# Two of three matrix products by Strassen's scheme, four stages with DRAM between them, cosine by half angle

## The chip, the cores and the metric

One core of a Trainium2 chip runs the whole program. The metric is the device time of one execution in microseconds (us), median of several runs. Every operand is float32. A product at near float32 precision is made of three TensorE passes over rounded operands (type float32r): high by high, high by low, low by high, where "low" is what the rounding of "high" left over.

## The reference, cut to what matters

```python
B, H, S, D = 4, 8, 768, 64        # 3072 tokens of 8 x 64 = 512 values
# attention: chunks of 32 queries; keys: 8 memory rows, 16 left, 32 own, 8 right
scores = (q_c @ k_full.T) / 8;  a = softmax(scores);  out_c = a @ v_full
x = out as [3072, 512]
h = x @ w_in                      # [512, 2048]
x = (h * cos(h)) @ w_out          # [2048, 512]
h = max(x @ w1, x @ w2, x @ w3)   # each [512, 768]
result = h @ w_out2               # [768, 512]
```

## The kernel before, in words

Attention runs on 24 subblocks of 128 tokens. For one of them TensorE makes the scores (L324, 16 small matmuls), VectorE subtracts the maximum (L616, L620), ScalarE takes the exponential of three subblocks at once (L486, after a load of its function table), TensorE turns the probabilities (L337), ScalarE copies them out (L493), TensorE multiplies with the values (L350), VectorE divides by the sum (L643), TensorE turns the result (L358), and ScalarE and VectorE write its high and low part (L497, L649).

The two expert layers run on 8 blocks of 384 tokens. **Stage 1** does attention, first product, cosine and second product together. For each of 16 slices f of the 2048 hidden features, `hidden` makes 12 matmuls of 384 columns (4 slices of 128 inputs, 3 passes), and `second` adds the slice that lies three behind it (LAG) into the output, 12 matmuls more. The attention of the next block stands between them by a fixed rule on f (`attend`). Between the products a slice is copied out of PSUM and turned into an angle on ScalarE (L504, L506), reduced to the range of the sine on VectorE (L662, L668, L677), passed through the sine on ScalarE (L512), multiplied and split in high and low on VectorE (L665, L674, L680). All weights of the stage stay in SBUF: POOL loads them once (L282) and subtracts for the low part (L287), after ScalarE rounded the high part (L531). The result goes to DRAM (`y_dram`), 768 KB a block.

**Stage 2** reads it back (L522, L690 for high and low), and for 6 slices of 128 features makes three products of 12 matmuls (`branch`), takes the largest of the three (L594, L755, L758), splits it (L764, L766), and `project` multiplies by the last matrix: 9 matmuls of 512 columns, summed over the 6 slices.

In numbers: 1536 + 1536 + 1728 matmuls of 384 columns and 432 of 512 columns. Each engine runs its own list in order, semaphores tie the lists together, and steady blocks are hardware loops (`blocks`). The loads of the attention come from SP's queue into one buffer for queries and keys and one for values: each load waits until the matmuls of the subblock before have read the buffer (L184).

Of the kernel before, what the change touches and what calls it, by code (L numbers as in the profile page):

```python
# [5 lines left out]
F32 = mybir.dt.float32  # L6
F32R = mybir.dt.float32r
I32 = mybir.dt.int32
# [8 lines left out]
P = 128  # L17
SUB = 128
NCH = SUB // CH
PAIRS = H // 2  # L20
BLK = 384
NSUB = BLK // SUB
NBLK = B * S // BLK
SUBS = B * S // SUB
# [9 lines left out]
LAG = 3  # L34
AHEAD = 3
WARM = 8
WSLOTS2 = NM * (NB2 + 1) // 2


PI = 3.141592653589793  # L40
ROUND = 1.5 * 2.0 ** 23
GONE = -3.0e38


def program(nc, qk_in, v_in, w1_in, w2_in, y_dram, out):
    ctx = ExitStack()
    with ctx:
# [6 lines left out]

        wts = sb("wts", [P, NF, 2, 2, 512], F32R)

        xh = sb("xh", [P, 2, KT, BLK], F32R)
        xl = sb("xl", [P, 2, KT, BLK], F32R)

        gh = sb("gh", [P, 4, BLK], F32R)  # L60
        gl = sb("gl", [P, 4, BLK], F32R)
        stage_and_tiles = sb("stage_and_tiles", [P, 8 * BLK])
        ostage = stage_and_tiles[:, 0:4 * BLK]
        tiles = stage_and_tiles[:, 4 * BLK:8 * BLK]
        hid = tiles[:, 0:2 * BLK].rearrange("p (b t) -> p b t", b=2)
        ang = tiles[:, 2 * BLK:4 * BLK].rearrange("p (b t) -> p b t", b=2)

        qk = sb("qk", [P, PAIRS * (2 * KC + SUB)])  # L70
        vals = sb("vals", [P, PAIRS * 2 * KC])
        prob = sb("prob", [P, NSUB, PAIRS, 2, KEYS])
        prob_t = sb("prob_t", [P, PAIRS, SUB])
        onat = sb("onat", [P, PAIRS, 2, D])
# [4 lines left out]
        wraw = sb("wraw", [P, 2, 2, 512])  # L79
        ident = sb("ident", [P, P])  # L80
        half_pi = sb("half_pi", [P, 1])
# [3 lines left out]
        yout = ostage[:, :].rearrange("p (m t) -> p m t", m=KT)  # L85
        ofin = ostage[:, 0:NSUB * DM].rearrange("p (i n) -> p i n", i=NSUB)
        yin = qk[:, 0:KT * BLK].rearrange("p (m t) -> p m t", m=KT)

        spare = stage_and_tiles[:, 0:PAIRS * (2 * KC + SUB)]

        def qk_at(t, j):
            b = spare if (t is T0 and j == 1) else qk[:, :]
            return b.rearrange("p (a x) -> p a x", a=PAIRS)

        def queries(t, j):
            return qk_at(t, j)[:, :, KC:KC + SUB]

        def keys(t, j, a, c):  # L100

            return two_parts(qk_at(t, j), a, c, KC + SUB)

        def vals_at(t, j):


            return (spare if (t is T0 and j == 1) else vals[:, :]).rearrange("p (a x) -> p a x", a=PAIRS)

        def head1_at(t, j):
            return KC + SUB if (t is T0 and j == 1) else KC  # L110

        def values_in(t, j, a, c):
            return two_parts(vals_at(t, j), a, c, head1_at(t, j))
# [6 lines left out]
        ps = ctx.enter_context(nc.psum_tensor("ps", [P, 8, 512], F32))  # L120
        T0 = 0
        HB = (4, 5)
        WB = (6, 7, 4, 5)

        def scores(t, j):
            return ps[:, (7, 5, 1)[j] if t is T0 else 7, :].rearrange("p (a r k) -> p a r k", a=PAIRS, r=2)

        def turned(t, j):
            return ps[:, (6, 4, 0)[j] if t is T0 else 6, :].rearrange("p (a t) -> p a t", a=PAIRS)

        def weighted(t, j):
            return ps[:, (7, 5, 1)[j] if t is T0 else 7, :].rearrange("p (a r d) -> p a r d", a=PAIRS, r=2)

        def inputs_at(n):


            return 32 * n

        def block_at(t):

            return t + NSUB

        qk_landed, v_landed = sem("qk_landed"), sem("v_landed")
        qk1_landed, v1_landed, zeroed = sem("qk1_landed"), sem("v1_landed"), sem("zeroed")
        w_landed = [sem("w_landed0"), sem("w_landed1")]
        w_high, w_ready = sem("w_high"), sem("w_ready")
        const_ready, const_base = sem("const_ready"), sem("const_base")
        qk_done, edge_masked, max_done, shifted = sem("qk_done"), sem("edge_masked"), sem("max_done"), sem("shifted")
# [4 lines left out]
        h_done, h_copied, turns_done = sem("h_done"), sem("h_copied"), sem("turns_done")  # L153
        k_done, r_done, abs_done, cos_done = sem("k_done"), sem("r_done"), sem("abs_done"), sem("cos_done")
        g_done, gh_done, g_ready, y_done = sem("g_done"), sem("gh_done"), sem("g_ready"), sem("y_done")
        y_out_act, y_out_dve, y_stored, y_landed = sem("y_out_act"), sem("y_out_dve"), sem("y_stored"), sem("y_landed")
        yh_ready, y_ready = sem("yh_ready"), sem("y_ready")
        br_done, first_copied, second_maxed, third_maxed = (
            sem("br_done"), sem("first_copied"), sem("second_maxed"), sem("third_maxed"))
        mh_done, m_ready, o_done = sem("mh_done"), sem("m_ready"), sem("o_done")  # L160
        fin_act, fin_dve, out_stored = sem("fin_act"), sem("fin_dve"), sem("out_stored")
# [4 lines left out]

        def blocks(eng, one):

            one(0, 0, True, False)
            with eng.Fori(0, (NBLK - 2) // 2) as i:  # L170
                one(2 * i + 1, 1, False, False)
                one(2 * i + 2, 0, False, False)
            one(NBLK - 1, (NBLK - 1) % 2, False, True)


        @block.sync
        def _(sp):


            def split_load(src, buffer, n, columns, landed):  # L180

                for r in range(2):
                    rows = slice(P // 2 * r, P // 2 * (r + 1))
                    sp.dma_start(buffer[rows, :, columns[r]],  # L184
                                 src[bass.ds(n, 1), rows, :].rearrange("n p (a x) -> (n p) a x", a=PAIRS))\
                      .then_inc(landed, 16)

            QK_COLUMNS = (slice(0, KC + SUB), slice(KC, 2 * KC + SUB))

            def v_columns(t, j):  # L190
                return (slice(0, KC), slice(head1_at(t, j), head1_at(t, j) + KC))

            def load_qk(n):
                sp.wait_ge(qk_done, n)
                sp.wait_ge(const_ready, 1)
                split_load(qk_in, qk_at(None, 0), n, QK_COLUMNS, qk_landed)

            def load_v(n):
                sp.wait_ge(pv_done, n)
                sp.wait_ge(const_ready, 1)  # L200
                split_load(v_in, vals_at(None, 0), n, v_columns(None, 0), v_landed)

            def store_y(t):

                sp.wait_ge(y_out_act, 2 * t + 2)
                sp.wait_ge(y_out_dve, 2 * t + 2)
                sp.wait_ge(const_ready, 1)
                sp.dma_start(y_dram[bass.ds(t, 1), :, :].rearrange("n p c -> (n p) c"), ostage).then_inc(y_stored, 16)
# [12 lines left out]

            def loads1(t, more, store):


                n = NSUB * t
                for j in range(1, NSUB + more):
                    load_qk(n + j)
# [591 lines left out]
```

## Time and profile before

| | |
|---|---|
| median of 3 runs | 1081.99 us (1080.62 to 1083.03) |
| span of the profiled execution | 1079.6 us |
| TensorE matmuls busy | 1032.5 us, 96% |
| VectorE, ScalarE, GpSimd busy | 538.5, 330.7, 83.6 us |
| DMA | 66.05 MB, mean 61 GB/s |
| mean granted TensorE clock | 0.983 of full speed |

The span runs from the first to the last instruction, the device time some 2 us longer. The durations of matmuls overlap, so that the distance between two starts, and not the duration, tells what one costs. Stage 1 lasts until some 680 us, stage 2 from there on.

### The profile page before, as it was taken

The numbers are of one execution on the slowest core, as the hardware profiler recorded it, in microseconds if no ns is written. First come the engines' busy times: TensorE is split into PE (matmuls) and PEld (weight loads), VectorE is DVE, ScalarE is ACT, GpSimd is POOL, SyncE is SP. The second block draws the span as 40 slices with busy tenths as digits, with TensorE's granted clock in tenths as the row PEclk, the third lists the DMA queues.
The fourth block names the chain that finished last, engine by engine and source line by source line (L and its number), as shares of the span: only waits on it lengthen the run. The fifth ranks groups of instructions, "written<-read, shape, count | busy, mean of one in ns | idle before, by whom it ended". The sixth has DMA issues, their size and how long they took to land.

```text
span 1079.6 us, 17509 instructions
## 1 busy us (share of the span) xinstructions
PE 1032.5 (96%) x6976; PEld 984.1 (91%) x6976; DVE 538.5 (50%) x1132; ACT 330.7 (31%) x575; POOL 83.6 (8%) x64
## 2 busy tenths in 40 slices
PE   5797999999999999999999977999999999999998
PEld 4687999999999999999999976999999999999997
DVE  5576665665665666665665666323222322233222
ACT  2455354344353353353443443101110101101000
POOL 1554000000000000000000354000000000000000
PEclk7699999999999999999999999999999999999999
DMA  8743231241321321311320231201010000000000
GB/s 212 183 143 117 69 89 40 52 107 30 73 77 40 89 49 42 101 39 40 89 59 11 70 97 59 85 4 59 3 58 30 29 29 29 29 29 29 0 30 30
DMA packets 35722, 66.05 MB, mean 61 GB/s; under 512 B 2368, under 2 KB 26944, under 8 KB 35648
## 3 DMA queue, kind: packets, MB, share of 16 engines
q1 hardware_dynamic: 31616, 50.34, 16.9%
q0 software_dynamic: 4032, 14.68, 4.2%
q8 instruction: 52, 0.85, 0.3%
q14 instruction: 22, 0.18, 0.1%
HBM read 52.43 MB, written 12.58 MB: 60 GB/s over the span
## 4 chain that ended last, share of the span: by engine, by line
PE 84%; DVE 8%; ACT 5%; DMA 2%; issue 1%; SPq 0%; ACTq 0%; DVEq 0%
PE ps L305 23%; PE ps L307 23%; PE ps L306 23%; DVE stage_and_tiles L662 3%; PE ps L461 3%; PE ps L462 3%; PE ps L460 3%; PE ps L350 2%; PE ps L324 2%; ACT wts L531 2%; DMA qk<-qk_in 1%; DVE stage_and_tiles L668 1%; ACT stage_and_tiles L506 1%; PE ps L358 1%; ACT stage_and_tiles L504 1%
## 5 line engine op out<-in xcount | busy, mean ns | idle before, releaser
L305 PE MATMUL ps<-xh,wts 128*128 128x384 f32 x1088 | 375.2, 345 | 3.1 <-issue 1.7
L307 PE MATMUL ps<-xh,wts 128*128 128x384 f32 x1088 | 366.6, 337 | 0.0
L306 PE MATMUL ps<-xl,wts 128*128 128x384 f32 x1088 | 365.9, 336 | 0.0
L305 PEld LDWEIGHTS ps<-xh,wts 128*128 128x128 f32 x1088 | 205.8, 189 | 14.7 <-issue 10.8
L306 PEld LDWEIGHTS ps<-xl,wts 128*128 128x128 f32 x1088 | 206.1, 189 | 2.0
L307 PEld LDWEIGHTS ps<-xh,wts 128*128 128x128 f32 x1088 | 205.7, 189 | 0.0
L305 PE MATMUL ps<-gh,wts 128*128 128x384 f32 x512 | 172.2, 336 | 13.1 <-DVE gl L680 12.8
L662 DVE TENSOR_SCALAR stage_and_tiles<-stage_and_tiles 128x384 f32<-128x384 f32 x128 | 76.6, 598 | 212.8 <-ACT stage_and_tiles L506 212.8
L307 PE MATMUL ps<-gh,wts 128*128 128x384 f32 x512 | 171.4, 335 | 0.0
L306 PE MATMUL ps<-gl,wts 128*128 128x384 f32 x512 | 171.1, 334 | 0.0
L512 ACT ACTIVATE stage_and_tiles<-stage_and_tiles,half_pi 128x384 f32<-128x384 f32 x128 | 79.0, 617 | 237.2 <-DVE stage_and_tiles L677 237.1
L755 DVE TENSOR_TENSOR stage_and_tiles<-stage_and_tiles,ps 128x384 f32<-128x384 f32 x48 | 26.6, 554 | 201.3 <-PE ps L307 201.3
L594 ACT COPY stage_and_tiles<-ps 128x384 f32<-128x384 f32 x48 | 23.1, 482 | 305.5 <-PE ps L307 305.5
L305 PEld LDWEIGHTS ps<-gh,wts 128*128 128x128 f32 x512 | 96.2, 188 | 16.6 <-DVE gl L680 16.0
L287 POOL TENSOR_TENSOR wts<-wraw,wts 128x1024 fp32r<-128x1024 f32 x28 | 66.7, 2381 | 566.5 <-ACT wts L531 566.5
L306 PEld LDWEIGHTS ps<-gl,wts 128*128 128x128 f32 x512 | 96.1, 188 | 0.0
L307 PEld LDWEIGHTS ps<-gh,wts 128*128 128x128 f32 x512 | 96.1, 188 | 0.0
L504 ACT COPY stage_and_tiles<-ps 128x384 f32<-128x384 f32 x128 | 61.3, 479 | 102.6 <-PE ps L307 102.6
L506 ACT ACTIVATE stage_and_tiles<-ps,rounder 128x384 f32<-128x384 f32 x128 | 75.0, 586 | 0.0
L665 DVE TENSOR_TENSOR stage_and_tiles<-stage_and_tiles 128x384 f32<-128x384 f32 x128 | 70.4, 550 | 0.2 <-ACT stage_and_tiles L512 0.2
L668 DVE SCALAR_TENSOR_TENSOR stage_and_tiles<-stage_and_tiles 128x384 f32<-128x384 f32 x128 | 70.4, 550 | 0.0
L680 DVE TENSOR_TENSOR gl<-stage_and_tiles,gh 128x384 fp32r<-128x384 f32 x128 | 70.3, 550 | 0.0
(63 smaller groups left out, 828.3 us busy)
## 6 DMA issues: line engine op xcount, KB each, us to landing
qk<-qk_in SPq DMA_DIRECT2D x46, 384.0 KB, 5.1
wraw<-w_in POOLq DMA_DIRECT2D x28, 512.0 KB, 3.7
vals<-v_in SPq DMA_DIRECT2D x46, 256.0 KB, 3.8
y_dram<-stage_and_tiles SPq DMA_DIRECT2D x8, 768.0 KB, 6.3
qk<-y_dram SPq DMA_DIRECT2D x8, 768.0 KB, 4.3
out<-stage_and_tiles SPq DMA_DIRECT2D x8, 768.0 KB, 3.6
stage_and_tiles<-qk_in SPq DMA_DIRECT2D x2, 384.0 KB, 9.2
stage_and_tiles<-v_in SPq DMA_DIRECT2D x2, 256.0 KB, 6.2
```

What stands on the lines that cost most here:

```text
L287: pool.tensor_tensor(wts[:, s, :, 1, :], wraw[:, g % 2, :, :], wts[:, s, :, 0, :].bitcast(F32), ALU.subtract).then_inc(w_ready, 1)
L305: pe.matmul(o, wh, mh, start=start, stop=False)
L306: pe.matmul(o, wh, ml, start=False, stop=False)
L307: return pe.matmul(o, wl, mh, start=False, stop=stop)
L460: pe.matmul(o, gh[:, m % 3, toks], w[:, 0, :], start=(m == 0), stop=False)
L504: act.copy(hid[:, f % 2, :], ps[:, HB[f % 2], 0:BLK]).then_inc(h_copied, 1)
L506: act.activation(ang[:, f % 2, :], ps[:, HB[f % 2], 0:BLK], ACT.Identity, scale=1.0 / (2 * PI), bias=rounder[:, :]).then_inc(turns_done, 1)
L512: act.activation(a, a, ACT.Sin, scale=-1.0, bias=half_pi[:, :]).then_inc(cos_done, 1)
L662: dve.tensor_scalar(a, a, ROUND, None, ALU.subtract).then_inc(k_done, 1)
L665: dve.tensor_tensor(hp, hp, ap, ALU.mult).then_inc(g_done, 1)
L668: dve.scalar_tensor_tensor(out=a, in0=a, scalar=-2 * PI, in1=hid[:, f % 2, :], op0=ALU.mult, op1=ALU.add).then_inc(r_done, 1)
L680: dve.tensor_tensor(glp, hp, ghp.bitcast(F32), ALU.subtract).then_inc(g_ready, 1)
```

## The change

**Stages.** Stage 1 becomes two. In the first (here A) are attention and `hidden` only, in blocks of 384 tokens; the gated result g goes to DRAM (`g_dram`, 16 slices by 3072 tokens). In the second (B) g comes back and is multiplied by `w_out`. Stage 2 becomes two as well: the three products with their maximum, written to DRAM (C), and the last product (D).

**Strassen's scheme** (Winograd's form) in B, C and D: both operands are cut in four quarters, and 7 products of sums of quarters take the place of 8. The sums (4 subtractions or additions per operand and unit) are made from the unrounded quarters, and all 7 combinations are rounded and split in high and low. A unit of B (48 of them: 6 token blocks of 512, 8 pairs of feature slices) is 7 products of 2 x 3 = 6 matmuls of 256 columns. For it VectorE makes four sums of 256 columns (`sums_g`), ScalarE rounds 7 x 256 = 1792 columns (`high_g`), and VectorE subtracts 1792 columns (`low_g`). At the end of a block of 8 units VectorE joins the 7 products by 7 additions of 512 columns. A unit of C (36) is 42 matmuls of 384 columns; a unit of D (12) is 63 of 256 columns. D's other operand, the 18 groups h, is prepared like g.

**Cosine.** With u = h/2pi and r = round(u) - u, h cos h = 2pi u (1 - 2 sin²(pi r)). ScalarE now makes copy, angle, sine and square of two slices at once (768 columns), VectorE two operations (`turn`, `gated`). The factor -2pi goes into `w_out`.

**Buffers.** The whole program is written out, without loops. B's g has 2 raw buffers and 3 prepared ones. Queries and keys, and values, keep one buffer each in the steady blocks.

The diff, cut to its core:

```diff
-                    if f >= LAG:
-                        second(t, f - LAG, first)
+        def attend(t, f):
+            n = NSUB * (t + 1)
...
+                if f == 1:
+                    scores_of(n + 1)
+                elif f == 3:
+                    scores_of(n + 2)
+                elif f == 6:
+                    turn_probs(n)
...
+                elif f == 10:
+                    values(n + 1)
+                    turn_out(n)
+                elif f == 11:
+                    values(n + 2)
...
+                elif f == 15 and t < NBLK - 2:
+                    scores_of(n + NSUB)
...
+            for n in range(UNITS1):
+                b, i = divmod(n, FPAIRS)
+                pe.wait_ge(g_ready, n + 1)
...
+                g, w = operand(9 + n % 3), operand(i)
+                for p in ORDER1:
...
+            def evacuate(i):
...
+                act.activation(hid(i), hidden_banks(i), ACT.Copy, scale=1.0 / (2 * PI)).then_inc(u_copied, 1)
...
+                act.activation(ang(i), hidden_banks(i), ACT.Identity, scale=1.0 / (2 * PI), bias=rounder[:, :])\
...
+            def cosine(i):
+                act.wait_ge(r_done, i + 1)
+                act.activation(ang(i), ang(i), ACT.Sin, scale=BELOW_PI).then_inc(sin_done, 1)
+                act.wait_ge(sin_done, i + 1)
+                act.activation(ang(i), ang(i), ACT.Square, scale=ROOT_TWO).then_inc(square_done, 1)
...
+            for t in range(NBLK):
...
+                for f in range(NF):
...
+                    if f % 2:
+                        i = FPAIRS * t + f // 2
+                        evacuate(i)
+                        if i:
+                            cosine(i - 1)
...
+                        if f == 5:
+                            exps(0, NSUB, n + NSUB)
...
+            def sums_cols(r, done, base):
+                dve.tensor_tensor(r[:, 4, :], r[:, 1, :], r[:, 0, :], ALU.subtract).then_inc(done, 1)
+                dve.wait_ge(done, base + 1)
...
+                if n and n + 2 < UNITS1:
+                    sums_g(n + 2)
+                if i == FPAIRS - 1:
...
+                    dve.tensor_tensor(y12, y11, ps[:, BANK1[6], :], ALU.add).then_inc(u2_done, 1)
...
+                if n and n + 2 < UNITS1:
+                    low_g(n + 2)
...
+            for n in range(UNITS1):
+                if n % FPAIRS == 0 and n:
+                    store_y(n // FPAIRS - 1)
...
+                if n >= 2 and n + 2 < UNITS1:
+                    load_g(n + 2)
...
+HIGH_H = (32, 33, 34, 35, 36, 37, 38, 38, 39, 40, 40, 41, 42, 42, 43, 44, 44, 45)
...
+                if 1 <= n <= 7:
+                    low_w2(n + 1)
...
+                for r in range(HUNITS):
+                    if HIGH_H[r] == n:
+                        sums_h(r)
+                for r in range(HUNITS):
+                    if HIGH_H[r] == n:
+                        low_h(r)
```

In the last lines n is the unit of C and D that TensorE works on; ScalarE's list has `high_w2(n + 1)` and `high_h(r)` at the same places. TensorE's list for a unit is products 1, 5, 7 (of the unit before), 2, 6, 3, 4 (of the unit before).

**Where instructions move, first place:** ScalarE in the first block, around the exponential of the attention. Before (`stage_and_tiles` holds the copied slice and the angle):

```order
L504 COPY stage_and_tiles<-ps 128x384
L506 ACTIVATE stage_and_tiles<-ps,rounder 128x384
L486 ACT_TABLE_LOAD
L486 ACTIVATE prob<-prob 128x1536
L512 ACT_TABLE_LOAD
L512 ACTIVATE stage_and_tiles<-stage_and_tiles,half_pi 128x384
```

And after, in the second block (`work` holds the slices, the angles and the probabilities):

```order
L805 ACTIVATE work<-ps 128x768
L808 ACTIVATE work<-ps,rounder 128x768
L813 ACTIVATE work<-work 128x768
L815 ACTIVATE work<-work 128x768
L784 ACT_TABLE_LOAD
L784 ACTIVATE work<-work 128x1536
L790 COPY prob_turned<-ps 128x512
```

The exponential now stands behind the sine and the square of the slice pair before.

**Second place:** VectorE in the second product. Before, for one slice:

```order
L662 TENSOR_SCALAR stage_and_tiles<-stage_and_tiles 128x384
L665 TENSOR_TENSOR stage_and_tiles<-stage_and_tiles 128x384
L668 SCALAR_TENSOR_TENSOR stage_and_tiles<-stage_and_tiles 128x384
L674 CAST gh<-stage_and_tiles 128x384
L677 TENSOR_SCALAR stage_and_tiles<-stage_and_tiles 128x384
L680 TENSOR_TENSOR gl<-stage_and_tiles,gh 128x384
```

After, the last unit of a block of B (`work` is the raw g and the sums of the result, `units` the prepared operands; L1084 to L1090 are `sums_g`, L1099 is `low_g`):

```order
L1084 TENSOR_TENSOR work<-work 128x256
L1086 TENSOR_TENSOR work<-work 128x256
L1088 TENSOR_TENSOR work<-work 128x256
L1090 TENSOR_TENSOR work<-work 128x256
L1228 TENSOR_TENSOR work<-work,ps 128x512
L1231 TENSOR_TENSOR work<-work,ps 128x512
L1099 TENSOR_TENSOR units<-work,units 128x1792
L1236 TENSOR_TENSOR work<-work,ps 128x512
L1238 TENSOR_TENSOR work<-work 128x512
L1240 TENSOR_TENSOR work<-work 128x512
L1243 TENSOR_TENSOR work<-work,ps 128x512
L1246 TENSOR_TENSOR work<-work,ps 128x512
```

In the other units the four sums stand directly ahead of `low_g`, which waits for ScalarE's `high_g` of the same unit, and that waits for the sums.

**Third place:** VectorE in the last product. Before, for one slice of the hidden features, it had this:

```order
L755 TENSOR_TENSOR stage_and_tiles<-stage_and_tiles,ps 128x384
L758 TENSOR_TENSOR stage_and_tiles<-stage_and_tiles,ps 128x384
L764 CAST gh<-stage_and_tiles 128x384
L766 TENSOR_TENSOR gl<-stage_and_tiles,gh 128x384
```

After, one unit of D (L1278 `c22` of the unit before, L1294 `c11`, L1299 `c12`), with two groups of h behind it:

```order
L1278 TENSOR_TENSOR work<-work,ps 128x256
L1294 TENSOR_TENSOR work<-work,ps 128x256
L1299 TENSOR_TENSOR work<-work,ps 128x256
L1132 TENSOR_TENSOR work<-work 128x256
L1134 TENSOR_TENSOR work<-work 128x256
L1136 TENSOR_TENSOR work<-work 128x256
L1138 TENSOR_TENSOR work<-work 128x256
L1132 TENSOR_TENSOR work<-work 128x256
L1134 TENSOR_TENSOR work<-work 128x256
L1136 TENSOR_TENSOR work<-work 128x256
L1138 TENSOR_TENSOR work<-work 128x256
L1143 TENSOR_TENSOR units<-work,units 128x1792 x2
```

All of it stands behind `c12`, which waits for product 3, the last but one of the unit.

## Rows read from the trace of the kernel before

**Rows 1.** The page: busy time of TensorE and of its weight loads.
```profile
PE 1032.5 (96%) x6976; PEld 984.1 (91%) x6976; DVE 538.5 (50%) x1132; ACT 330.7 (31%) x575; POOL 83.6 (8%) x64
```

**Rows 2.** Stretches: us, busy (count) of PE, PEld, DVE, ACT, POOL, clock, DMA share, GB/s.
```profile
640.00:680.00 40.00, 32.15 (x178) 30.23 (x177) 24.99 (x41) 14.05 (x25) 16.65 (x10) 1.00 0.17 56
800.00:900.00 100.00, 100.00 (x541) 95.29 (x540) 29.03 (x52) 10.68 (x18) 0.00 (x0) 1.00 0.09 31
```

**Rows 3.** Chain of waits, 200 to 400 us: the first scores of two neighbouring blocks.
```profile
281.40 1.01 PE ps L324 x32
...
358.04 1.01 PE ps L324 x32
```

**Rows 4.** TensorE over time in stage 2: start, duration, line; 19 and 9 matmuls apart.
```profile
799.79 0.33 PE L307 MATMUL ps<-xh,wts 128*128 128x384 f32 x1
...
803.09 0.39 PE L460 MATMUL ps<-wts,gh 128*128 128x512 f32 x1
...
805.17 0.33 PE L305 MATMUL ps<-xh,wts 128*128 128x384 f32 x1
```

**Rows 5.** Four turns of 128 columns and the matmul after, all engines over time.
```profile
309.72 0.53 PEld L337 LDWEIGHTS ps<-ident,prob 128*128 128x128 f32 x4
309.89 0.60 PE L337 MATMUL ps<-ident,prob 128*128 128x128 f32 x4
...
310.25 0.42 PE L305 MATMUL ps<-xh,wts 128*128 128x384 f32 x1
```

**Rows 6.** Groups by form: VectorE and ScalarE by width; busy us, mean ns, idle before.
```profile
L306 PEld LDWEIGHTS ps<-gl,wts 128*128 128x128 f32 x512 | 96.1, 188 | 0.0
...
L512 ACT ACTIVATE stage_and_tiles<-stage_and_tiles,half_pi 128x384 f32<-128x384 f32 x128 | 79.0, 617 | 237.2 <-DVE stage_and_tiles L677 237.1
...
L665 DVE TENSOR_TENSOR stage_and_tiles<-stage_and_tiles 128x384 f32<-128x384 f32 x128 | 70.4, 550 | 0.2 <-ACT stage_and_tiles L512 0.2
...
L504 ACT COPY stage_and_tiles<-ps 128x384 f32<-128x384 f32 x128 | 61.3, 479 | 102.6 <-PE ps L307 102.6
...
L690 DVE TENSOR_TENSOR xl<-qk,xh 128x1536 fp32r<-128x1536 f32 x8 | 15.0, 1869 | 2.5 <-ACT xh L522 2.5
...
L522 ACT CAST xh<-qk 128x1536 fp32r<-128x1536 f32 x8 | 11.8, 1481 | 0.0
...
L486 ACT ACTIVATE prob<-prob 128x1536 f32<-128x1536 f32 x7 | 10.4, 1488 | 0.1
L512 ACT ACT_TABLE_LOAD x8 | 10.3, 1283 | 0.1
```

**Rows 7.** VectorE over time in stage 2: an operation and the one that waits for it.
```profile
803.28 0.56 DVE L758 TENSOR_TENSOR stage_and_tiles<-stage_and_tiles,ps 128x384 f32<-128x384 f32 x1 [1.44 <-PE ps L307]
803.87 0.36 DVE L764 CAST gh<-stage_and_tiles 128x384 fp32r<-128x384 f32 x1
```

**Rows 8.** The page's DMA issues: line, count, size, us from issue to landing.
```profile
qk<-qk_in SPq DMA_DIRECT2D x46, 384.0 KB, 5.1
wraw<-w_in POOLq DMA_DIRECT2D x28, 512.0 KB, 3.7
vals<-v_in SPq DMA_DIRECT2D x46, 256.0 KB, 3.8
y_dram<-stage_and_tiles SPq DMA_DIRECT2D x8, 768.0 KB, 6.3
qk<-y_dram SPq DMA_DIRECT2D x8, 768.0 KB, 4.3
```

**Rows 9.** SP's queue over time: the two issues of one load of queries and keys.
```profile
292.16 1.26 SPq L184 DMA_DIRECT2D qk<-qk_in  x2
```

**Rows 10.** TensorE over time, first block: first `hidden`, and a stop of 4.00 us.
```profile
33.62 0.69 PE L305 MATMUL ps<-xh,wts 128*128 128x384 f32 x1 [1.40 <-DVE xl L649]
...
83.25 1.11 PE L358 MATMUL ps<-ident,onat 128*128 128x128 f32 x4 [4.00 <-DVE onat L643]
```

**Rows 11.** A stretch, TensorE alone: us, busy (count), clock, DMA share, GB/s.
```profile
82.00:86.00 4.00, 2.75 (x10) 0.66 0.31 115
```

More of the change, by code:

```diff
@@ L52, in sem, with sems @@
             return ctx.enter_context(nc.semaphore(name))
[L55 to L74, printed above, removed]
+        def sems(name, n):
+            return [sem(f"{name}{i}") for i in range(n)]
+        work = sb("work", [P, 11776])
         smax = sb("smax", [P, NSUB, PAIRS, 2])
@@ L157, in program @@
[L157 to L161, printed above, removed]
-        block = ctx.enter_context(nc.Block())
[L167 to L173, printed above, removed]
+        h_done, u_copied, turns_done = sem("h_done"), sem("u_copied"), sem("turns_done")
@@ new lines, in qk_sem, with v_sem, pieces @@
+        def qk_sem(n):
+            return (qk_landed[n], 32) if n < NSUB else (qk_landed[3], 32 * (n - NSUB + 1))
+        def v_sem(n):
+            return (v_landed[n], 32) if n < NSUB else (v_landed[3], 32 * (n - NSUB + 1))
+        def pieces(first, n, width):
+            at = 0
+            while at < n:
+                t, off = (first + at) // width, (first + at) % width
+                m = min(width - off, n - at)
+                yield t, off, at, m
+                at += m
+        Y_PIECES = [sum(2 * len(list(pieces(2 * HALF * b + HALF * j, HALF, BLK))) for j in range(2))
+                    for b in range(NBLK1)]
@@ new lines, in load_v2 @@
+            def load_v2(v):
+                if v == 0:
+                    pool.wait_ge(w2_ready, UNITS)
+                else:
+                    pool.wait_ge(y_ready, 7 * NBLK2)
+                for half in range(2):
+                    unit = (NB2 + 1) * (2 * v + half) + NB2
+                    pool.dma_start(raw_d[v][:, 2 * half:2 * half + 2, :],
+                                   w2_in[unit // 2, :, 512 * (unit % 2):512 * (unit % 2) + 512]
+                                   .rearrange("p (q c) -> p q c", q=2)).then_inc(v2_landed, 16)
@@ L465, in block2 @@
-            def block2(t, parity, first, last):
-                for m in range(NM):
-                    for j in range(NB2):
-                        branch(t, parity, m, j, first)
-                        if first and m == 0:
-                            second(NBLK - 1, NF - LAG + j, False)
-                    if m:
-                        project(t, m - 1, first)
-                    elif not first:
-                        project(t - 1, NM - 1, False)
-            blocks(pe, block2)
-            project(NBLK - 1, NM - 1, False)
+                pe.matmul(ps[:, 7, 0:P], ident[:, :], ident[:, :], start=True, stop=True)
```

1434 lines of the change are left out of this document (976 added, 458 removed).

## The prediction

> **What bounds the kernel now.** I read the page first: TensorE is busy 96% [rows 1]. The stretches say how steady that is: all of 800 to 900 us, and 80% of 640 to 680, at full clock in both [rows 2]. So TensorE sets the pace, and the question for the change is whether it still does. The time lines give what a matmul costs: 384 columns take (803.09 - 799.79) / 19 = 0.1737 us, 512 columns (805.17 - 803.09) / 9 = 0.2311 us [rows 4], both 0.452 ns per column. From one block's first scores to the next are 76.6 us [rows 3]; 384 matmuls take 66.6 of it, the attention's own matmuls with the pauses around them 10.1 (about 1.2 for scores or values, 0.5 for a turn). The rows by form give VectorE and ScalarE as a start-up and a rate: a two-operand VectorE operation goes from 550 to 1869 ns between 384 and 1536 columns, so 1.145 ns per column: 0.40 us for 256, 0.69 for 512, 0.99 for 768, 2.16 for 1792; a ScalarE copy goes from 479 to 1481 ns, 0.87 per column: 1.70 us for 1792 [rows 6]. A dependent operation starts 0.03 us after the end of the one it waits for [rows 7].
>
> **What TensorE gains.** The 1536 matmuls of the second product become 2016 of 256 columns, the 1728 of the branches 1512 of 384, the 432 of the last product 756 of 256: together 184,320 columns fewer, 83 us at 0.452 ns. A matmul of 256 columns isn't in the trace. The low end is 0.1157 us, columns alone. The high end: four turns of 128 columns, each with a weight load of its own, take 310.25 - 309.89 = 0.36 us, 0.090 each, 0.032 above the columns' 0.058 [rows 5]; with that added it is 0.148. I take the low end, since 384 and 512 columns show no fixed part. Before, the products' matmuls make 4800 x 0.1737 + 432 x 0.2311 = 934 us; the rest is attention, start and stops. If nothing else changed this would be the forecast. But the sums and splits that pay for the scheme lie on VectorE and ScalarE, and their order makes them serial. I go stage by stage.
>
> **Stage A** (attention and first product). *Start:* 33.6 us before [rows 10]; the loads are no longer held back by the matmuls, 31. *A steady block* has 192 x 0.1737 = 33.3 us of product and 10.1 of attention. What hid the attention's waits was the second product, which doubled the distance of its steps. Four stops come back. (1) The exponential: ScalarE reaches it behind copy (0.81) and angle, sine and square (0.95 each) of 768 columns (479 and 617 ns plus 384 x 0.87 [rows 6]), 3.4 us with their overlap, then a table load of 1.28 and 1.49 itself: 6.2 us after f = 5, where TensorE has one f of 2.1 us: 4.1 stopped. (2) and (3) The single buffer of queries and keys: 1.3 us of issue [rows 9], the second half 5.1 to land [rows 8], so 5.8 us from one scores to the next, against two f, 4.2 us: 1.6, twice. (4) Values: 0.7 + 3.8 [rows 8] against a turn and one f, 2.6: 1.9. Together 43.4 + 9.2 = 52.6. Starts of five blocks have 2.1 more, since the subtraction of a weight group (1792 columns, 2.2 us) stands ahead of `shift` on VectorE. A stop of 4.0 us was followed by a stretch at 0.66 of the clock: 0.34 x 4 = 1.4 us lost [rows 10, 11]; I add 1.5 to 2.5 per block for the stop of 4.1. Six blocks: 6 x 52.6 + 5 x 2.1 + 6 x 2.2 = 340. The first has slow clock and weight splits in ScalarE's list, 62. The last has no attention: 33.3, and ScalarE with 8 x 3.4 + 4 x 1.7 = 34, 38. The store of g must land before the third pair after it is copied out: 4.5 us to the gated result, 0.7 issue, 3.7 landing (taken from the 512 KB load of rows 8), 8.9 per two pairs: 4.4 per pair against 4.2, no more than grazed. Ends: 3.7 or 6.3 (the y_dram store), the latter 50 us per stage. **A: 31 + 62 + 340 + 38 = 471.**
>
> **Stage B** (second product). TensorE needs 42 x 0.1157 = 4.86 us per unit. VectorE's list is four dependent sums, 4 x (0.40 + 0.03) = 1.75; then it waits 1.70 + 0.04 for ScalarE's rounding; then 2.16 + 0.03 for the low part; nothing stands between, and the next unit's sums come behind. That is 5.7 us per unit, so VectorE's order sets the pace, whatever the three prepared buffers allow. The load (4.3 to land at most [rows 8], while two buffers leave 5.7) is hidden in it. 45 units behind the three prepared in A: 257. Five block ends: the copy of product 1 behind `high_g` (0.6), two joins in front of `low_g` (1.45), five behind (3.6): 5.7 each, 28. After each, SP first issues 4 to 6 stores of the result, the last of which waits for the last join, and only then the load that VectorE's next sums need: about 1.2 us until its issue, 4.3 to land, 1 to 2 behind 1 MB of stores: 7 to 8 us each, 39 with the extra load at block 5. The last two weight groups and one of C: 8; lead-in behind A's last cosine: 9; y of stage C (four sums, seven splits, some in the shadow): 9; last unit 5. **B: 355,** against 1536 x 0.1737 = 267 for the same product before. At the high matmul price TensorE would need 6.2 per unit: 24 more.
>
> **Stage C** (branches). 1512 x 0.1737 = 262. In its first eight units the next unit's weights are split at the end of ScalarE's and VectorE's lists. ScalarE rounds them (1.70) after its copy of product 6, which ends 1.6 us before the unit does, or, in units 1, 4 and 7, after the copy of product 4, 0.5 after the end; VectorE then subtracts (2.16), not before product 4's maximum. TensorE waits 4.4 us three times and 2.8 four times: 25. The first four groups h: 1.75 + 1.74 + 2.19 + 3.7 for the joins is 9.4 per unit against 7.3: 8. New y in three blocks 2, clock 5. **C: 302.**
>
> **Stage D** (last product). 756 x 0.1157 = 87. The third group h that a pair of units needs is prepared behind `c12` of the unit just before (at 37, 39, 41, 43, 45): from 0.6 us before its end 5.7 us, so 5.1 stopped, and two groups in one list (7.9 us) hold the joins back so that product 4 waits 1.5 in four units: 26 + 6. Clock 8, last store and joins 7. **D: 134,** against 432 x 0.2311 = 100.
>
> Sum 471 + 355 + 302 + 134 = 1262 of span, to be set against 1079.6; the median lies 2.4 above the span, so 1264 us.
>
> **Range.** Known costs with unknown overlap: A ±25 (a stop more or less of 1.5 us in 30 places), the 256-column price up to +24 in B and 756 x 0.032 = +24 in D, the reload after a block's end 0 to 12 us, 5 times, stops in C and D half hidden -30. 1180 to 1345.
>
> **Rivals.** *TensorE keeps the pace* (the other side). If sums, rounding and subtraction were hidden, as they are where an engine runs ahead by a buffer, it would be A 31 + 51 (43.4 and 8 for the slow clock of the start) + 6 x 43.4 + 33 = 375, B 233 + 9, C 262, D 87 + 7: 975 us. It decides where preparing a unit takes under 4.86 us. For it: VectorE's busy time alone per unit, 1.6 + 2.2 = 3.8, is less. Against it: the list of VectorE has no other work between sums and `low_g`, and 1.7 us of rounding on ScalarE lie between them. With stage B alone hidden it is still 1262 - 355 + 242 = 1149, slower. *Stores of g as slow as y_dram's 6.3*: 5.8 us per pair in A where no stop covers it, up to 50 more: 1310. *Weight loads come to light at 256 columns*: a load is recorded with 188 ns [rows 6]; were that the least distance of two matmuls, a unit of B would take 7.9 us and one of D 11.8: B 48 x 7.9 + 67 = 446, D 12 x 11.8 + 30 = 172, together 129 more: near 1390. Against it: the four turns' loads have 0.53 us between them and pass in 0.36 [rows 5]. The Trainium skill ("TensorE: Matmul & The Clock Gate", section "LDWEIGHTS (loading the stationary operand)") has a load take its columns over 1.2 GHz, 107 ns for 128; an estimate by that page, with nothing of it hidden, is 0.22 us for 256 columns and 9.4 us for a unit of B. By that rule alone the turns would be no closer than 107 ns, and the trace has 90. *The clock falls for good* in B, to its lower level of 1.2 GHz: a unit at twice the price, 9.7 us, and 180 us more; 80% busy at a clock of 1.00 [rows 2] speaks against it, since B would be 4.86 / 5.7 = 85% busy. *Other, smaller:* half of A's stops absent and B's list shorter, 1085 to 1180.
>
> **Chances.** Forecast 0.77; slow stores 0.07 (in the range for the most part); loads or clock 0.05; the smaller 0.05; TensorE-paced or near it 0.06, of which 0.01 by the old time. 0.77 + 0.07 + 0.05 + 0.05 + 0.06 = 1; the range holds the first two and lets go of 0.16 to 0.2 in all. A measurement of this kernel can tell 0.2% (2 us) from no change: slower 0.94, within 0.2% 0.01, faster 0.05.
>
> **What would show it.** In the profile after, B: `low_g` (1792 columns) near 2.16 us with VectorE idle 1.7 before it, released by ScalarE; TensorE's matmuls waiting for `low_g` once per unit; unit distance 5.7; 256 columns 0.116 apart. A: TensorE waiting for the exponential once a block, some 4 us, and for queries and keys twice; block distance 53 to 57. C: seven waits for the weights' low part. D: five waits of 5 us for h. The forecast is wrong if TensorE is over 90% busy in B, or A's blocks are under 48 us.

## The result and the profile after

The changed kernel takes 1262.8 us (median of 4 runs, 1255.8 to 1268.9) against 1082.5: 1.167 times as long, 95% interval 1.162 to 1.171. Forecast were 1264 us and a range of 1180 to 1345. The page of the changed kernel, its span, busy times, the clock by slices and the chain that ended last:

```profile
span 1259.6 us, 18304 instructions
...
PE 1037.5 (82%) x7564; PEld 997.0 (79%) x7564; DVE 686.4 (54%) x926; ACT 512.6 (41%) x641; POOL 156.4 (12%) x199
...
PEclk6998989899989999989898897989899999998888
...
PE 41%; DVE 25%; ACT 15%; DMA 11%; issue 6%; SPq 2%; DVEq 0%; ACTq 0%
```

Against [rows 1] TensorE is busy 82% of a longer span, for about the same time (1037.5 and 1032.5 us): it has fewer columns, but some of them at the lower clock. On the chain of work that ended last TensorE had 84% before (the page's chain line) and has 41% now: VectorE, ScalarE and DMA set the end at least as much.

The stretches of the changed kernel, cut where the first `hidden` starts and where the width of the matmuls changes, in the columns of [rows 2]: start, A, B, C, D.

```profile
0.00:36.89 36.89, 21.70 (x265) 17.34 (x265) 15.06 (x27) 8.59 (x15) 13.94 (x23) 0.63 0.84 179
36.89:480.90 444.01, 365.28 (x3017) 340.92 (x3017) 219.70 (x279) 269.12 (x334) 78.62 (x100) 0.93 0.46 132
480.90:818.43 337.53, 269.66 (x2017) 264.65 (x2017) 218.02 (x293) 100.53 (x76) 15.14 (x19) 0.91 0.32 100
818.43:1118.40 299.97, 272.04 (x1502) 268.36 (x1501) 162.07 (x214) 92.41 (x154) 48.71 (x58) 0.97 0.21 75
1118.40:1259.60 141.20, 108.78 (x769) 105.69 (x768) 71.58 (x117) 42.00 (x63) 0.00 (x0) 0.87 0.30 99
```

| stage | forecast | measured |
|---|---|---|
| start and A | 471 | 480.9 |
| B | 355 | 337.5 |
| C | 302 | 300.0 |
| D | 134 | 141.2 |
| span | 1262 | 1259.6 |

What TensorE waited for, longest in total first (times, longest one), in the changed kernel:

```profile
PE ps L546 <- DVE units L1099: 44.7, 15, 8.5
...
PE ps L573 <- ACT work L784: 28.1, 7, 4.0
PE ps L546 <- DVE units L1105: 26.0, 7, 4.8
PE ps L546 <- DVE units L1143: 24.7, 5, 5.0
PE ps L546 <- ACT work L938: 20.0, 5, 4.2
PE ps L587 <- DMA work<-v_in: 19.6, 9, 3.4
PE ps L562 <- DMA work<-qk_in: 18.2, 10, 2.3
PE ps L562 <- DVE work L1023: 14.6, 5, 3.2
```

L1099 is the low part of g (B), L784 the exponential (A), L1105 the weights' low part (C), L1143 the low part of h (D), L938 the copy of product 1 at a block's end of B, then the loads of values and of queries and keys and `shift` (VectorE's subtraction of the maximum) in A. The counts are the forecast's: seven exponentials, seven weights, five h. In B TensorE doesn't wait once per unit: it is idle for 67.9 us, nearly all in the two long rows of B (44.7 and 20.0) and five waits of 0.6 us for a join, and most of it at the ends of blocks. The other 31 us above its 2016 matmuls at 0.1185 us are matmuls further apart than that, at a mean clock of 0.91. The chain that ended last, in B alone, shows what sets the pace; VectorE has half of it and TensorE almost nothing:

```profile
by line: DVE units L1099 26.5%; ACT units L831 19.8%; DMA work<-g_dram 7.4%; DVE work L1090 5.9%; DVE work L1088 5.9%; DVE work L1086 5.9%; issue 5.8%; DVE work L1084 5.0%; SPq L318 1.7%; PE ps L546 1.2%; PE ps L547 1.2%; DVE units L1080 1.
```

VectorE over time in B, the end of a block and then a unit at the start of the next one:

```profile
528.55 2.02 DVE L1099 TENSOR_TENSOR units<-work,units 128x1792 fp32r<-128x1792 f32 x1 [1.76 <-ACT units L831]
530.50 0.42 DVE L1084 TENSOR_TENSOR work<-work 128x256 f32<-128x256 f32 x1
...
531.87 0.42 DVE L1090 TENSOR_TENSOR work<-work 128x256 f32<-128x256 f32 x1
534.60 0.69 DVE L1228 TENSOR_TENSOR work<-work,ps 128x512 f32<-128x512 f32 x1 [2.31 <-ACT work L938]
...
540.33 0.68 DVE L1246 TENSOR_TENSOR work<-work,ps 128x512 f32<-128x512 f32 x1
546.67 0.42 DVE L1084 TENSOR_TENSOR work<-work 128x256 f32<-128x256 f32 x1 [5.67 <-DMA work<-g_dram]
...
548.05 0.42 DVE L1090 TENSOR_TENSOR work<-work 128x256 f32<-128x256 f32 x1
550.22 2.02 DVE L1099 TENSOR_TENSOR units<-work,units 128x1792 fp32r<-128x1792 f32 x1 [1.75 <-ACT units L831]
552.16 0.42 DVE L1084 TENSOR_TENSOR work<-work 128x256 f32<-128x256 f32 x1
```

Four sums, 1.75 us of idleness while ScalarE rounds, the subtraction, and the next unit: 552.16 - 546.67 = 5.49 us. At the end of a block come the joins, and then 5.67 us until the late load of g has landed. This list, with its block ends, takes some 54.5 us for 8 units. TensorE needs 5.0 us a unit at full clock, catches up within a block, and waits at its end: for the copy of product 1, which stands in ScalarE's list behind the rounding that waits for VectorE's sums, and then for the first `low_g` of the new block.

### The profile page after: what moved, and what is told of

It is laid out like the page before. It is cut to its first block, busy times and chain, and to the rows that moved or that the text cites. A ratio compares the mean times of both kernels' runs of the same rounds, so it can differ in the third digit from the quotient of the medians.

```text
span 1259.6 us, 18304 instructions
## 1 busy us (share of the span) xinstructions
PE 1037.5 (82%) x7564; PEld 997.0 (79%) x7564; DVE 686.4 (54%) x926; ACT 512.6 (41%) x641; POOL 156.4 (12%) x199
## 4 chain that ended last, share of the span: by engine, by line
PE 41%; DVE 25%; ACT 15%; DMA 11%; issue 6%; SPq 2%; DVEq 0%; ACTq 0%
PE ps L546 12%; PE ps L548 12%; PE ps L547 12%; DVE units L1099 7%; ACT units L831 5%; DMA work<-qk_in 4%; DMA work<-v_in 3%; DMA work<-g_dram 2%; PE ps L587 2%; PE ps L562 2%; DVE work L1088 2%; DVE work L1086 2%; DVE work L1090 2%; ACT work L808 1%; DVE units L1143 1%
## 5 line engine op out<-in xcount | busy, mean ns | idle before, releaser
L546 PE MATMUL ps<-units 128*128 128x384 f32 (+1 forms) x1940 | 644.1, 332 | 124.9 <-DVE units L1099 44.7
L547 PE MATMUL ps<-units 128*128 128x384 f32 (+1 forms) x1940 | 628.6, 324 | 0.0
L548 PE MATMUL ps<-units 128*128 128x384 f32 (+1 forms) x1940 | 627.9, 324 | 0.0
L546 PEld LDWEIGHTS ps<-units 128*128 128x128 f32 x1940 | 394.1, 203 | 144.7 <-issue 83.4
L547 PEld LDWEIGHTS ps<-units 128*128 128x128 f32 x1940 | 394.1, 203 | 0.0
L548 PEld LDWEIGHTS ps<-units 128*128 128x128 f32 x1940 | 393.0, 203 | 0.0
L831 ACT CAST units<-work 128x1792 fp32r<-128x1792 f32 x48 | 80.9, 1686 | 233.8 <-DVE work L1090 233.8
L965 ACT COPY work<-ps 128x384 f32<-128x384 f32 (+1 forms) x144 | 63.6, 453 | 221.3 <-PE ps L548 221.3
L1058 DVE SCALAR_TENSOR_TENSOR work<-work 128x768 f32<-128x768 f32 x64 | 62.7, 980 | 148.1 <-ACT work L808 148.1
L1099 DVE TENSOR_TENSOR units<-work,units 128x1792 fp32r<-128x1792 f32 x48 | 97.1, 2023 | 70.1 <-ACT units L831 70.1
L805 ACT ACTIVATE work<-ps 128x768 f32<-128x768 f32 x64 | 51.8, 809 | 130.9 <-PE ps L548 130.2
L1278 DVE TENSOR_TENSOR work<-work,ps 128x384 f32<-128x384 f32 (+1 forms) x48 | 24.9, 519 | 115.5 <-PE ps L548 115.5
L1063 DVE SCALAR_TENSOR_TENSOR work<-work 128x768 f32<-128x768 f32 x64 | 61.9, 968 | 42.0 <-ACT work L815 41.9
L808 ACT ACTIVATE work<-ps,rounder 128x768 f32<-128x768 f32 x64 | 57.3, 896 | 1.6 <-DVE work L1063 1.6
L815 ACT ACTIVATE work<-work 128x768 f32<-128x768 f32 x64 | 54.1, 845 | 2.0
L813 ACT ACTIVATE work<-work 128x768 f32<-128x768 f32 x64 | 54.0, 844 | 0.1
L1143 DVE TENSOR_TENSOR units<-work,units 128x1792 fp32r<-128x1792 f32 x18 | 36.1, 2024 | 17.7 <-ACT units L871 17.5
L1299 DVE TENSOR_TENSOR work<-work,ps 128x384 f32<-128x384 f32 (+1 forms) x48 | 24.9, 519 | 35.8 <-PE ps L548 35.7
```

Of the source, the lines that this page charges most:

```text
L546: pe.matmul(o, wh, mh, start=start, stop=False, skip_group_check=onto)
L547: pe.matmul(o, wh, ml, start=False, stop=False, skip_group_check=onto)
L548: return pe.matmul(o, wl, mh, start=False, stop=stop, skip_group_check=onto)
L808: act.activation(ang(i), hidden_banks(i), ACT.Identity, scale=1.0 / (2 * PI), bias=rounder[:, :])\
L813: act.activation(ang(i), ang(i), ACT.Sin, scale=BELOW_PI).then_inc(sin_done, 1)
L815: act.activation(ang(i), ang(i), ACT.Square, scale=ROOT_TWO).then_inc(square_done, 1)
```

## The experiments

Each edits the changed kernel; the medians stand beside runs of the kernel before on the same chip (1082.1 to 1082.5), and the differences are to the changed kernel's 1262.8. The stretches have the columns of [rows 2].

**e1_split: rounding and subtraction of g in two pieces.**

```diff
-                act.wait_ge(g_sums, 4 * n + 4)
+                act.wait_ge(g_sums, 4 * n + 2)
...
-                act.copy(operand(9 + n % 3)[:, 0, :, :], graw[n % 2]).then_inc(g_high, 1)
+                act.copy(g[:, 0, 0:5, :], graw[n % 2][:, 0:5, :]).then_inc(g_high, 1)
+                act.wait_ge(g_sums, 4 * n + 4)
+                act.copy(g[:, 0, 5:7, :], graw[n % 2][:, 5:7, :]).then_inc(g_high, 1)
```

> Stage B only: ScalarE rounds g in two pieces, 1280 columns after the second of the four sums and 512 after the fourth, and VectorE subtracts in the same two pieces. If the serial list sums, rounding, subtraction sets the pace of B (5.49 us per unit in the trace of the changed kernel), the list falls to about 4.3 us and TensorE's 42 x 0.1157 = 4.86 takes over: 45 x 0.63 = 28 us less, some 3 us more at the block ends, about 1232 us. If TensorE's waits in B come from the loads of g, the opening of the banks or a matmul that costs more than its columns, at most 5 us less.

1208.3 us, ratio 1.116 (1.111 to 1.121): 54 less. B, and two subtractions of first pieces in VectorE's list where nothing holds it:

```profile
476.99:768.28 291.29, 257.80 (x2018) 254.21 (x2018) 222.53 (x341) 105.50 (x123) 13.41 (x19) 0.94 0.37 118
```

```profile
583.76 1.49 DVE L1102 TENSOR_TENSOR units<-work,units 128x1280 fp32r<-128x1280 f32 x1 [0.40 <-ACT units L832]
...
587.98 1.49 DVE L1102 TENSOR_TENSOR units<-work,units 128x1280 fp32r<-128x1280 f32 x1 [0.41 <-ACT units L832]
```

The list falls to 4.22 us with the same work in it (its idle time, not its operations, was the loss), and B by 46 us. The rivals named ahead of the run (loads of g, the opening of the banks, dearer matmuls) allowed 5 us, so the serial list is the cause. The gain in B is half as large again as the 31 us expected. Most of TensorE's stops for the copy of product 1 went with it (20.0 to 2.5 us), and those for `low_g` fell from 44.7 to 27.4; the clock rises from 0.91 to 0.94. The late load stays: VectorE still waits 34.4 us for g.

**e2_store: the load of g ahead of the stores at a block's start.**

```diff
+                if n >= 2 and n + 2 < UNITS1:
+                    load_g(n + 2)
                 if n % FPAIRS == 0 and n:
                     store_y(n // FPAIRS - 1)
...
-                if n >= 2 and n + 2 < UNITS1:
-                    load_g(n + 2)
```

> Stage B only: at a block's start SP issues the load of g ahead of the stores of the block before. If the load of g stands too late behind the last join and the store issues (VectorE waits 33.3 us for it in 6 places), VectorE's waits of about 5.7 us go and B is 25 to 32 us shorter: about 1233 us. If TensorE is held at a block's start by the opening of its banks (20 us of waits for the copies of product 1) and VectorE's wait lies in its shadow, under 8 us less.

1227.9 us, ratio 1.134 (1.133 to 1.136): 35 less.

```profile
477.41:786.90 309.49, 265.72 (x2018) 259.24 (x2017) 217.60 (x293) 100.60 (x76) 15.24 (x19) 0.93 0.35 109
```

VectorE's waits for g in B, 31.3 us in 5 places in the changed kernel, are nearly gone:

```profile
DVE work L1084 <- DMA work<-g_dram: 3.6, 2, 3.3
```

B became 28.0 us shorter by two statements put in another order. TensorE's waits for the copies of product 1 are unchanged (21.1 us in 5 places), so VectorE's wait did not lie in their shadow. They are a loss of their own, and e1_split is the edit that takes them away.

**e3_exp: the exponential ahead of the pair's copies in ScalarE's list.**

```diff
+                    if f == 5 and t < NBLK - 1:
+                        exps(0, NSUB, n + NSUB)
                     if f % 2:
                         i = FPAIRS * t + f // 2
                         evacuate(i)
```

> Stage A only: in ScalarE's list the exponential stands ahead of the copies of the pair f = 4, 5 instead of behind the sine and square. If the place in the list makes TensorE's stop (28.1 us in 7 places), it goes, and the clock lost behind it too: 28 to 40 us less, about 1225 us. If ScalarE's load as a whole makes the stop (269 of 444 us busy in A), it comes back at the next pair's copies: under 10 us less.

1240.2 us, ratio 1.146 (1.144 to 1.148): 23 less, of which A gave 17.2. The start gave most of the rest: with the same code it took 32 to 37 us in these profiled executions. TensorE's waits in A:

```profile
PE ps L587 <- DMA work<-v_in: 25.9, 13, 3.3
PE ps L562 <- DMA work<-qk_in: 15.4, 9, 2.5
PE ps L562 <- DVE work L1023: 14.7, 5, 3.2
PE ps L573 <- issue: 7.6, 7, 1.9
```

The 28.1 us for the exponential are gone, so their place in the list made them. But the gain is below the 28 to 40 us expected: 6.3 us went over to the loads of values (19.6 before), and the clock in A rose only from 0.93 to 0.94. The last row, 7.6 us, is a new stop and not a rest of the old one: it is the turn of the second subblock, and e9_best shows below what it waits for. The expectation had left out what comes behind the stop it removed.

**e4_h: the third group h one unit earlier.**

```diff
-HIGH_H = (32, 33, 34, 35, 36, 37, 38, 38, 39, 40, 40, 41, 42, 42, 43, 44, 44, 45)
+HIGH_H = (32, 33, 34, 35, 36, 36, 37, 38, 38, 39, 40, 40, 41, 42, 42, 43, 44, 44)
```

> Stage D only: the third group h of a pair of units is prepared one unit earlier (another table HIGH_H). If the preparation at the end of the unit just before makes TensorE's five stops (24.7 us), they go, and waits for the joins behind two groups in one list stay or grow by 1 us each: 15 to 28 us less with the clock, about 1240 us. If VectorE as a whole is the limit of D (14 groups at 5.5 us and 12 x 1.2 us of joins are 91 us of 141), the stops only move to the joins: under 8 us less.

1220.8 us, ratio 1.125 (1.121 to 1.130): 42 less.

```profile
1113.36:1218.60 105.24, 95.77 (x769) 93.44 (x768) 70.71 (x117) 41.24 (x63) 0.00 (x0) 1.00 0.39 132
```

D falls from 141.2 to 105.2 us. VectorE does the same work (71 us), so its load as a whole was no limit. 24.7 us are the stops; the other 11 come with the clock, 0.87 before and 1.00 now.

**e5_w2: the weights of C rounded and subtracted in mid-unit** (ScalarE ahead of the copy of product 6, VectorE ahead of the join c12).

```diff
+                    if 1 <= n <= 7:
+                        high_w2(n + 1)
                     snap(n, 6, bank_b(n), snap6, c12_done, n, s6_copied)
...
+                if 1 <= n <= 7:
+                    low_w2(n + 1)
                 if n < UNITS_ALL:
                     c12(n)
```

> Stage C only: in its first eight units the next unit's weights are rounded ahead of the copy of product 6 and subtracted ahead of the join c12, instead of at the ends of both lists. If the place in the lists makes TensorE's seven stops (26.0 us), they go: 22 to 30 us less, about 1235 us. If the weights come late from POOL (its sums of 256 columns take 0.7 to 1.5 us each, and two raw buffers) ScalarE and VectorE now wait earlier and hold the joins: under 8 us less, or slower.

1223.0 us, ratio 1.130 (1.126 to 1.133): 40 less.

```profile
814.58:1081.91 267.33, 262.64 (x1502) 259.58 (x1501) 161.59 (x214) 92.86 (x154) 49.48 (x58) 1.00 0.24 85
```

C falls from 300.0 to 267.3 us, within 5 of its 1512 matmuls at 0.1737 us. Of the 26.0 us of stops 2.4 are left, in 5 short waits; 23.6 went, and the other 9 go with the clock (0.97 to 1.00). The rival, weights that come late from POOL, would have left most of it.

**e7_space: e3_exp, and the attention's steps wider apart** (scores at f = 14, 1, 4, values at 8, 10, 12; `shift` moves with the scores, and that of the next block's first subblock to f = 15, ahead of the weights' subtraction at the block's start; the turns and splits of the result one slice later).

```diff
-                    elif f == 3:
+                    elif f == 4:
                         scores_of(n + 2)
...
-                    elif f == 11:
+                    elif f == 12:
                         values(n + 2)
```

> Stage A only: the exponential ahead of the pair's copies as in e3_exp, and the attention's steps set wider: scores at f = 14, 1, 4 (three slices apart), values at 8, 10, 12. If the single buffers and the 5.8 us from one load to the next make the rest of A's stops (15.8 us for queries and keys, 19.6 for values, 14.6 behind the weights' subtraction), most of these go too, 30 to 45 us beyond e3_exp, with the clock: about 1185 us. If the loads are slowed by the stores of g on the same 16 DMA engines (132 GB/s in A), they stay late at the wider distance: under 12 us beyond e3_exp.

1214.4 us, ratio 1.121 (1.118 to 1.123): 48 less than the changed kernel, 26 less than e3_exp.

```profile
35.25:438.87 403.62, 353.62 (x3017) 328.29 (x3018) 218.80 (x279) 267.81 (x335) 78.87 (x100) 0.96 0.51 145
```

A falls by 40 against the changed kernel and by 23 against e3_exp. In A the waits for queries and keys go from 15.8 to 5.2 us, for values from 19.6 to 12.2, and those behind `shift` are gone; 17.1 us appear in 7 turns of the result (L596), which now stand behind VectorE's work on the sine, and 13.6 in front of the second subblock's turn of the probabilities (7.6 in e3_exp). So the distance of two slices, too short for one buffer and one load, made most of the waits for queries and keys, and the stores of g don't make the loads too slow for three. Several things moved at once here, and a second buffer wasn't tried. The gain beyond e3_exp, 26 us, stayed below the 30 to 45 expected, since moved steps met another list.

**e6_all: e1 to e5 together, and h in two pieces like g.**

> The edits of e1_split, e2_store, e3_exp, e4_h and e5_w2 together, and h rounded in two pieces as g. If the stops are independent, the gains add: 28 + 28 + 33 + 22 + 25 = 136 us and some for h, about 1120 us, still slower than the kernel before. If one stop hides another, under 100 us less.

1094.2 us, ratio 1.010 (1.006 to 1.013): 169 less. C takes 265.6 us, and B:

```profile
461.41:724.34 262.93, 251.06 (x2018) 248.64 (x2017) 222.45 (x341) 105.64 (x123) 13.41 (x19) 0.97 0.42 130
```

The stops are independent, stage by stage: e1_split and e2_store alone took 46.2 and 28.0 us from B, and together 74.6. The medians of the singles give 54 + 35 + 23 + 42 + 40 = 194, more than 169, because each contains more than its stage: the start of the changed kernel, 36.9 us in its profiled execution, was 32 to 35 us in the others with the same code. Still 1% slower than the kernel before. The piece of the edit on h has no run of its own; D is 103.6 us against 105.2 in e4_h.

**e8_both: e6_all with the wider steps.**

> e6_all with the wider attention steps of e7_space. If the stops are what the scheme loses and TensorE then keeps the pace: A 37 + 7 x 46 + 38 = 397, B 245, C 266, D 100, about 1010 us of span and faster than the kernel before by some 6%. If A's loads or ScalarE's load bound it instead: 1070 to 1100 us.

1069.0 us, ratio 0.986 (0.983 to 0.989): 1.4% less than the kernel before, and 25 us less than e6_all.

```profile
35.38:436.79 401.41, 352.08 (x3017) 326.37 (x3018) 218.25 (x281) 267.89 (x337) 78.92 (x100) 0.97 0.51 146
436.79:700.62 263.83, 250.01 (x2018) 247.20 (x2017) 222.27 (x341) 105.40 (x122) 13.37 (x19) 0.98 0.41 130
```

Of the 59 us above what was expected A has 40 (437 with the start, against 397) and B 19 (264 against 245); C and D are as expected. A was taken too low as a whole: the waits of e7_space are all still there. 1069 is at the edge of the range given to the other reading, that A's loads or ScalarE's load bind it (1070 to 1100).

**e9_best: e8_both, scores at f = 13, 0, 3 and the second turn of the result at 12** (with VectorE's and ScalarE's steps that belong to them).

```diff
-                    if f == 1:
+                    if f == 0:
                         scores_of(n + 1)
-                    elif f == 4:
+                    elif f == 3:
                         scores_of(n + 2)
```

> e8_both with the scores one slice earlier (f = 13, 0, 3) and the second turn of the result back at f = 12. In e8_both TensorE still waits in A 13.8 us in 7 places for the exponential (scores end at f = 4, and 2 us are missing) and 17.1 us in 7 places for the turn that stands behind VectorE's sine work. If both are set by these places in the lists, A loses 20 to 30 us: about 1045 us, faster than the kernel before by some 3.5%. If ScalarE's and VectorE's lists in A are simply full (268 and 218 of 401 us busy, but in bursts), the waits move and it stays within 8 us of 1069.

1048.0 us, ratio 0.970 (0.967 to 0.973).

```profile
35.60:414.11 378.51, 344.39 (x3016) 319.38 (x3017) 218.27 (x281) 268.12 (x336) 78.97 (x100) 0.99 0.54 154
```

The median falls by 21 us and A by 23. The 17.1 us of the turns behind VectorE's list are gone, and values wait 7.7 us for 11.4; queries and keys wait 11.7 for 6.9. The 12.8 us that the expectation put down to the exponential stayed, so the missing 2 us of distance aren't their cause. The trace shows another. All engines over time:

```profile
209.75 0.60 PE L573 MATMUL ps<-ident,work 128*128 128x128 f32 x4
209.78 1.28 ACT L813 ACT_TABLE_LOAD   x1
...
212.70 0.57 ACT L790 COPY prob_turned<-ps 128x512 f32<-128x512 f32 x1
...
213.37 0.63 PE L573 MATMUL ps<-ident,work 128*128 128x128 f32 x4 [0.93 <-issue]
```

The first subblock's turn starts in time, so the exponential is there. It is the second turn that waits, for ScalarE's copy of the first one (L790), which stands in ScalarE's list behind the table load, the sine and the square of the pair. In all seven places the turn starts 0.1 us behind the end of that copy, and so it does in e3_exp. No run moved the copy.

## Why the prediction was right, step by step

**The pace of B** was the heart of it: VectorE's sums, ScalarE's rounding and VectorE's subtraction in series, 5.7 us per unit against TensorE's 4.86. Measured are 5.49 and, for the same work in another order, 4.22 (e1_split). The difference to 5.7 is one term: the subtraction of 1792 columns took 2.02 us where the line through 384 and 1536 columns gave 2.16, and the next sum, which doesn't depend on it, started 0.08 before its end and not 0.03 behind it. The other operations came out as priced (0.42 for 0.40, ScalarE's 1792 columns 1.69 for 1.70). 45 x 0.2 = 9 us of the 17 by which B was forecast too long; the late loads, 31.3 us at five block ends for 39, give 8 more.

One sign was wrong: TensorE was to wait for `low_g` once per unit, with units 5.7 us apart. The pace of 5.49 is that of VectorE's list. TensorE has 15 listed waits for `low_g` in 48 units, and the rest of its idle time at the block ends. The list as a whole does bound B, as the chain shows, but TensorE pays in lumps. Its 80% of busy time there is well under the 90% that would have spoken against the forecast.

**The price of 256 columns**: taken at 0.1157 us, between ends of 0.1157 and 0.148. TensorE over time at the start of B:

```profile
480.90 0.28 PE L546 MATMUL ps<-units 128*128 128x256 f32 x1
...
482.44 0.28 PE L547 MATMUL ps<-units 128*128 128x256 f32 x1
```

13 matmuls lie between: 0.1185 us, near the low end. The rival of exposed weight loads is out: the page records 0.203 us for a load on average, more than the distance between two starts, so loads and matmuls overlap. By the Trainium skill ("TensorE: Matmul & The Clock Gate", section "LDWEIGHTS (loading the stationary operand)") a load takes its columns over 1.2 GHz, 107 ns for 128. An estimate by that page for load and 256 columns in series is 0.22 us; the 0.1185 measured rules the series out.

**The stops of A.** The exponential: 4.1 us a block forecast, 28.1 / 7 = 4.0 measured. ScalarE over time in one block, and TensorE's turn behind it:

```profile
236.36 1.28 ACT L784 ACT_TABLE_LOAD   x1
237.65 1.48 ACT L784 ACTIVATE work<-work 128x1536 f32<-128x1536 f32 x1
```

```profile
239.19 1.11 PE L573 MATMUL ps<-ident,work 128*128 128x128 f32 x4 [4.01 <-ACT work L784]
```

Values: 13 us forecast, 19.6 measured. Queries and keys with the weights' subtraction: 6 x 3.2 + 10.5 = 30 forecast, 15.8 in A and 14.6 measured.

The blocks themselves came out worse than A's total says. The exponentials of neighbouring blocks (the table loads of L784, the first at 59.49 us, the seventh at 414.21) are 59.1 us apart on average, where the six steady blocks were forecast at 340 / 6 = 56.7, and most lie outside the 53 to 57 us that the prediction named as a sign. That is 15 us too short for the six; the first block and the last, forecast at 62 + 38 = 100, took the other 89 of A's 444.0 us, 11 too long. That the two nearly cancel is luck. Of the 15, the longer waits for values are some 6, and the clock is a part: the mean of 0.93 over 444 us is 31 us at most, since TensorE also waited while it was low, against 21 forecast for A. The rest was not taken apart. (The prediction also rounded: 384 x 0.1737 is 66.7 and not 66.6, which leaves 9.9 for the attention, 1 us over all of A.)

The start was 5.9 us later than forecast. The first subblocks ran at a clock of 0.63. With the same code the start took 33.1, 33.9 and 34.8 us in e2_store, e5_w2 and e1_split, at clocks of 0.79, 0.75 and 0.71: it follows the clock, and some 4 of the 5.9 us belong to this execution.

**The stops of C and D**: 25 and 26 us forecast, 26.0 and 24.7 measured, in seven and five places as counted. D is 7 us longer than forecast. The clock is 3 of them: 8 us forecast, and 11 by what e4_h gained beyond the stops. The price of 256 columns is 756 x 0.0028 = 2, and 12 matmuls of C's width that lie in this stretch are 2.

**Against the rivals.** *Stores of g as slow as y_dram's*: the page after has 3.6 us to landing for g_dram, as taken (3.7). *The clock falls for good* in B: its mean is 0.91. *TensorE keeps the pace*: only after the lists were set in another order, and then near 1048, not 975.

So the mechanisms held (serial lists, single buffers, late preparation), with TensorE's waits in B in other places than foreseen. That forecast and median lie 1 us apart is luck: start with A and D were 10 and 7 us too short, B and C 17 and 2 too long.

**Where the 83 us of saved columns went:** in e9_best, with most stops gone, 34 us of them arrive. Start and A take 414 us there, about what stage 1 took without its second product (some 680 - 267 = 413). B takes 262.7 us against 267 for that product, though its columns became 34 us cheaper. The old stage 2, some 400 us, became C and D with 265.6 + 103.6 = 369 us, and C has nearly all of the gain: its matmuls alone are 262.6 us. So what is lost lies in B (29 us above its columns at 0.1157) and D (16 above), not in A. In B, by its trace, it is the price of 0.1185 (6 us), some 12 us of listed waits, and for the rest matmuls further apart, at a mean clock of 0.97.

## What to carry to other kernels

A scheme that saves TensorE's columns must be priced by the list of the engine that prepares the operands, in its order: add up one unit with its waits (5.7 us forecast, 5.49 measured), not its busy time (3.8 forecast), add the ends of the blocks, and compare with TensorE's need. Where work is split in stages, look at what the removed stage was hiding: every wait that had two products' time now has one. Read a stage's pace from its chain and not from the waits of the engine that you care for, which can come in lumps far from their cause. And once such a kernel is slow, the cure may be cheap: six edits that only move statements or cut an operation in two took 169 us off.

## What the runs showed of the hardware beyond that

**A stop costs more than itself.** After a stop of 4.91 us in D TensorE started 24 matmuls of 256 columns over 5.26 us, most of them 0.213 us apart, at a granted clock of 0.50 (1.2 GHz), before it came back to 0.12:

```profile
1163.86 0.55 PE L546 MATMUL ps<-units 128*128 128x256 f32 x1 [4.91 <-DVE units L1143]
...
1164.64 0.41 PE L546 MATMUL ps<-units 128*128 128x256 f32 x1
...
1169.12 0.32 PE L546 MATMUL ps<-units 128*128 128x256 f32 x1
1169.28 0.28 PE L547 MATMUL ps<-units 128*128 128x256 f32 x1
1169.39 0.28 PE L548 MATMUL ps<-units 128*128 128x256 f32 x1
```

The 5.3 us at the lower level cost some 2.4 us here. In e4_h and e5_w2 the gains were 36.0 and 32.6 us in their stages for 24.7 and 23.6 us of stops that went: 1.46 and 1.38 times the stop.

**VectorE's additions in SBUF doubled beside POOL's.** While POOL summed weights in B (its four sums, one row here), VectorE's sum of 256 columns took 0.84 us, and 0.42 right after:

```profile
519.34 0.80 POOL L478 TENSOR_TENSOR work<-work 128x256 f32<-128x256 f32 x1
```

```profile
519.57 0.84 DVE L1088 TENSOR_TENSOR work<-work 128x256 f32<-128x256 f32 x1
...
525.45 0.42 DVE L1086 TENSOR_TENSOR work<-work 128x256 f32<-128x256 f32 x1
```

It is seen in this one stretch, not tested by a run; that moving sums to POOL doesn't relieve VectorE one for one is a warning, not a finding.
